# One table entry per round, the last one carried in a register, and the ring slot by modulo

## The reference

```python
# attention, per step t; x is y brought to (3072, 384)
y[t] = r[t] @ (state + (u * k[t]) outer v[t])
state = w[t][:, None] * state + k[t] outer v[t]
# layer 1: expert by normalised x against normalised expert_emb, over tau
# layer 2: expert by x @ w_gate, scaled also with sigmoid(x @ w_output_gate)
for e in range(8):
    mask = expert_idx == e
    h = np.maximum(x[mask] @ w1[e], 0.0)
    out[mask] = gate_w[mask, None] * (h @ w2[e])   # layer 2: times the output gate
```

## Time and profile before

| | |
|---|---|
| Runs | 804.28 us median of 3 (802.75 to 806.98) |
| Profiled execution | 805.82 us, of which the span is 804.1 us |
| Mean granted TensorE clock | 0.978 of full speed |
| PE busy | 734.2 us (91%) |
| PEld busy | 646.0 us (80%) |
| DVE busy | 503.9 us (63%) |
| ACT busy | 390.5 us (49%) |
| POOL busy | 161.2 us (20%) |
| HBM | 130 GB/s over the span |

### The profile page before, as it was taken

How to read it: one execution, slowest core, us unless ns; L and a number is a source line. 1 busy time by engine, 2 the same in 40 slices (tenths; PEclk the granted TensorE clock), 3 DMA queues, 4 the chain that set the end, 5 groups by cost and what they waited for, 6 DMA issues and landing times.

```text
span 804.1 us, 21458 instructions
## 1 busy us (share of the span) xinstructions
PE 734.2 (91%) x5566; PEld 646.0 (80%) x5567; DVE 503.9 (63%) x1363; ACT 390.5 (49%) x761; POOL 161.2 (20%) x202
## 2 busy tenths in 40 slices
PE   3898898883899999999999998799999999999994
PEld 2787776673788889888888887679999999999993
DVE  7889999987557574747575575544544444426621
ACT  3556767871445453636454563154444444425521
POOL 5444655554000000000000000000000000110000
PEclk9989999996999999999999999899999999999998
DMA  6655688634734251413353343233515252415110
GB/s 132 149 149 152 165 244 249 168 105 172 265 99 144 91 194 38 164 47 118 110 196 99 115 132 104 101 119 116 196 35 190 71 166 86 149 43 193 39 34 26
DMA packets 50269, 103.75 MB, mean 129 GB/s; under 512 B 7921, under 2 KB 29904, under 8 KB 50224
## 3 DMA queue, kind: packets, MB, share of 16 engines
q1 hardware_dynamic: 29536, 67.18, 26.9%
q10 hardware_dynamic: 15568, 21.76, 10.1%
q0 software_dynamic: 5120, 14.26, 4.9%
HBM read 85.73 MB, written 19.01 MB: 130 GB/s over the span
## 4 chain that ended last, share of the span: by engine, by line
PE 68%; DVE 11%; issue 7%; DMA 5%; ACT 4%; ACTq 3%; POOL 1%; SPq 1%; DVEq 0%; POOLq 0%
PE bank L1313 18%; PE bank L1339 17%; PE bank L1347 10%; PE bank L1318 9%; PE bank L1328 5%; DMA rk<-rk_in 2%; PE bank L1280 2%; PE bank L1302 2%; DVE Q L760 2%; DVE SF L769 2%; ACT wall L562 2%; PE bank L1129 1%; DMA sorted<-yrow,slot 1%; ACTq L507 1%; POOL rkp L394 1%
## 5 line engine op out<-in xcount | busy, mean ns | idle before, releaser
L1313 PE MATMUL bank<-wall,xT_hi 128*128 (+1 forms) x660 | 176.9, 403 | 1.3 <-ACT xT_hi L655 1.3
L1339 PE MATMUL bank<-wall,hT_hi 128*128 x880 | 166.9, 341 | 0.5 <-ACT hT_hi L664 0.5
L1339 PEld LDWEIGHTS bank<-wall,hT_hi 128*128 128x128 f32 x880 | 154.2, 189 | 7.9 <-issue 5.6
L875 DVE TENSOR_TENSOR wall<-raw,wall 128x1024 f32 (+1 forms) x96 | 111.9, 1220 | 62.2 <-ACT wall L562 58.9
L1313 PEld LDWEIGHTS bank<-wall,xT_hi 128*128 128x128 f32 x660 | 117.5, 188 | 21.1 <-issue 1.8
L659 ACT ACTIVATE hs<-bank 128x512 f32<-128x512 f32 x110 | 65.2, 592 | 106.7 <-PE bank L1318 106.7
L562 ACT ACTIVATE wall<-raw 128x1024 f32 (+1 forms) x96 | 95.1, 1050 | 42.4 <-issue 42.4
L664 ACT ACTIVATE hT_hi<-bank 128x512 fp32r<-128x512 f32 x110 | 59.8, 596 | 70.4 <-PE bank L1328 70.4
L1318 PE MATMUL bank<-wall,xT_lo 128*128 (+1 forms) x330 | 93.9, 392 | 0.0
L1347 PE MATMUL bank<-wall,hT_lo 128*128 x440 | 91.3, 349 | 0.0
L465 POOL DMA_INDIRECT sorted<-yrow,slot x28 | 27.4, 978 | 295.0 <-DVE yrow L1019 295.0
(11 more groups left out here) (198 smaller groups left out, 987.5 us busy)
## 6 DMA issues: line engine op xcount, KB each, us to landing
raw<-wall_in SPq DMA_DIRECT2D x96, 512.0 KB, 4.8
xin<-sorted ACTq DMA_DIRECT2D x59, 194.0 KB, 2.7
rk<-rk_in SPq DMA_DIRECT2D x46, 192.0 KB
v_in<-v_src ACTq DMA_DIRECT2D x24, 192.0 KB, 3.6
vT<-vT_in ACTq DMA_DIRECT2D x48, 96.0 KB, 4.7
wb<-w_in SPq DMA_DIRECT2D x46, 96.0 KB
sorted<-padrow SPq DMA_DIRECT2D x16, 194.0 KB, 2.3
sorted<-yrow,slot POOLq DMA_INDIRECT x28, 2.6
```

The lines of the kernel that those rows point to most:

```text
L875: v.tensor_tensor(w_lo[:, slot, cols], raw[:, q], w_hi[:, slot, cols].bitcast(F32), ALU.subtract).then_inc(w_split, 1)
L1313: pe.matmul(bank[n][:, :], xT_hi[:, k, :], w[:, bass.ds(slot, 1), cols].rearrange("p o n -> p (o n)"), start=(k == 0 and w is w_hi), stop= ...
L1339: pe.matmul(bank[2][:, 0:DM], hT_hi[:, j, :], w[:, bass.ds(slot, 1), W2 + j * DM:W2 + (j + 1) * DM].rearrange("p o n -> p (o n)"), start=( ...
```

## The change

`TAB_SLOT` and `TAB_PLACE` and the two instructions that fill them are dropped; the copy now writes the whole of `tab`. On PE the expert of tile p+1 is read once at the start of the turn and kept in the register `expert`, from which the next turn takes the expert of its tile p; the slot is the expert modulo `RING`. On ScalarE and VectorE the mark for p is read once in a turn (`following`) and kept in the register `begun`, from which the next turn takes the mark for its p-1; the place is the mark modulo `RING`. `snap` turns a register into a value that stays as it is when the register is written again, here with bounds given. The order of all other work is as it was.

```diff
@@ -50,9 +50,7 @@
 
 TAB_E, TAB_OFF, TAB_FIRST = 0, TT, 2 * TT
 TAB_LAST = TAB_FIRST + TT + 1
-TAB_SLOT = TAB_LAST + 1
-TAB_PLACE = TAB_SLOT + TT
-TAB = TAB_PLACE + TT + 1
+TAB = TAB_LAST + 1
 WRANGE = 0.25
 GT = 16
 EQ = D // 4
@@ -240,12 +238,13 @@
 
         SOON, LATE = range(3), range(3, RAWS)
 
-        def with_next_expert(eng, m, g, split, pieces):
-
-
-            e1 = eng.value_load(tab[0:1, m, bass.ds(g + TAB_FIRST + 1, 1)], min_val=0, max_val=E)
+        def following(eng, m, g):
+            return eng.value_load(tab[0:1, m, bass.ds(g + TAB_FIRST + 1, 1)], min_val=0, max_val=E)
+
+        def split_next(eng, m, g, e1, split, pieces):
+
             with eng.If(e1 > 0):
-                place = eng.value_load(tab[0:1, m, bass.ds(g + TAB_PLACE + 1, 1)], min_val=0, max_val=1)
+                place = eng.snap(e1 % RING, min_val=0, max_val=RING - 1)
                 eng.wait_ge(moes[m]["mm2"], g + 2)
                 for q in pieces:
                     split(E * m + e1, bass.ds(place, 1), q)
@@ -642,6 +641,7 @@
                 act.wait_ge(rts[1]["sel"], g)
                 act.activation(r1[:, 6:7], r1[:, 4:5], ACT.Exp, scale=-1.0).then_inc(rts[1]["ex"], 1)
 
+            begun = act.alloc_register("act_begun")
             for m in range(2):
                 mo = moes[m]
 
@@ -682,10 +682,13 @@
                     relu(0, n)
                 copy_xt(1)
                 load_rows(2)
+                act.reg_mov(begun, 0)
                 with act.Fori(0, last) as p:
                     copy_ht(p)
-                    with_next_expert(act, m, p - 1, split_hi, LATE)
-                    with_next_expert(act, m, p, split_hi, SOON)
+                    split_next(act, m, p - 1, act.snap(begun, min_val=0, max_val=E), split_hi, LATE)
+                    e1 = following(act, m, p)
+                    act.reg_mov(begun, e1)
+                    split_next(act, m, p, e1, split_hi, SOON)
                     if m == 0:
                         copy_yt(p + 1)
                         keep_row(p + 1)
@@ -697,16 +700,17 @@
                     load_rows(p + 3)
 
                 copy_ht(last)
-                with_next_expert(act, m, last - 1, split_hi, LATE)
+                split_next(act, m, last - 1, act.snap(begun, min_val=0, max_val=E), split_hi, LATE)
                 if m == 0:
-                    with_next_expert(act, m, last, split_hi, SOON)
+                    e1 = following(act, m, last)
+                    split_next(act, m, last, e1, split_hi, SOON)
                     copy_yt(last + 1)
                     keep_row(last + 1)
                     exps(last + 1)
                     copy_yt(last + 2)
                     keep_row(last + 2)
                     exps(last + 2)
-                    with_next_expert(act, m, last, split_hi, LATE)
+                    split_next(act, m, last, e1, split_hi, LATE)
 
                 act.wait_ge(mo["x_in"], 16 * last + 48)
                 part(act)
@@ -903,9 +907,7 @@
                                                 op0=ALU.is_lt, op1=ALU.mult))
                 link(v.scalar_tensor_tensor(out=FIRST, in0=NUM[:, 1:], scalar=1.0, in1=FIRST, op0=ALU.add, op1=ALU.mult))
                 link(v.tensor_scalar(tabf[:, TAB_LAST:TAB_LAST + 1], ends[:, E - 1:E], 1.0, None, ALU.subtract))
-                link(v.tensor_copy(tab[:, m, 0:TAB_SLOT], tabf[:, 0:TAB_SLOT]))
-                link(v.tensor_scalar(tab[:, m, TAB_SLOT:TAB_PLACE], tab[:, m, TAB_E:TAB_E + TT], 1, None, ALU.bitwise_and))
-                v.tensor_scalar(tab[:, m, TAB_PLACE:TAB], tab[:, m, TAB_FIRST:TAB_LAST], 1, None, ALU.bitwise_and).then_inc(tabs[m], 1)
+                v.tensor_copy(tab[:, m, :], tabf[:, :]).then_inc(tabs[m], 1)
 
             def first(u, b):
                 pre(u, b, lambda: None)
@@ -1027,6 +1029,7 @@
             link(v.tensor_copy(oha[:, 1, :], accbase[:, :]))
             v.sem_inc(r2["slots"], 1)
 
+            begun = v.alloc_register("dve_begun")
             for m in range(2):
                 mo = moes[m]
 
@@ -1066,10 +1069,13 @@
                 keep_ext(1)
                 rest_xt(1)
                 last = v.value_load(tab[0:1, m, TAB_LAST:TAB_LAST + 1], min_val=E - 1, max_val=TILES - 2)
+                v.reg_mov(begun, 0)
                 with v.Fori(0, last) as p:
                     rest_ht(p)
-                    with_next_expert(v, m, p - 1, split_lo, LATE)
-                    with_next_expert(v, m, p, split_lo, SOON)
+                    split_next(v, m, p - 1, v.snap(begun, min_val=0, max_val=E), split_lo, LATE)
+                    e1 = following(v, m, p)
+                    v.reg_mov(begun, e1)
+                    split_next(v, m, p, e1, split_lo, SOON)
                     if m == 0:
                         choose(p + 1)
                     keep_ext(p + 2)
@@ -1081,9 +1087,10 @@
                     gated(p)
 
                 rest_ht(last)
-                with_next_expert(v, m, last - 1, split_lo, LATE)
+                split_next(v, m, last - 1, v.snap(begun, min_val=0, max_val=E), split_lo, LATE)
                 if m == 0:
-                    with_next_expert(v, m, last, split_lo, SOON)
+                    e1 = following(v, m, last)
+                    split_next(v, m, last, e1, split_lo, SOON)
                     choose(last + 1)
                     place_row(last + 1)
                 v.wait_ge(mo["y_sb"], last + 1)
@@ -1096,7 +1103,7 @@
                     link(v.tensor_tensor(n_e, bank[3][:, 48:48 + E], ecap[:, :], ALU.subtract))
                     place_row(last + 2)
                     tables(1, link)
-                    with_next_expert(v, m, last, split_lo, LATE)
+                    split_next(v, m, last, e1, split_lo, LATE)
 
 
         @block.tensor
@@ -1289,12 +1296,12 @@
                     last = pe.matmul(bank[3][:, 48:48 + E], ones_r[:, :], acc, start=False, stop=True)
                 last.then_inc(r2["cnt"], 1)
 
+            expert = pe.alloc_register("pe_expert")
             for m in range(2):
                 mo = moes[m]
 
-                def weights(g):
-                    slot = pe.value_load(tab[0:1, m, bass.ds(g + TAB_SLOT, 1)], min_val=0, max_val=1)
-                    return slot, pe.value_load(tab[0:1, m, bass.ds(g + TAB_E, 1)], min_val=0, max_val=E - 1) * RAWS + E * RAWS * m
+                def weights(e):
+                    return pe.snap(e % RING, min_val=0, max_val=RING - 1), e * RAWS + E * RAWS * m
 
                 def transpose_x(g):
                     pe.wait_ge(mo["x_in"], 16 * g + 16)
@@ -1360,13 +1367,16 @@
                 pe.wait_ge(mo["xT_lo"], 1)
                 transpose_x(1)
                 last = pe.value_load(tab[0:1, m, TAB_LAST:TAB_LAST + 1], min_val=E - 1, max_val=TILES - 2)
+                pe.reg_mov(expert, 0)
                 with pe.Fori(0, last) as p:
-                    slot, pieces = weights(p + 1)
+                    old_slot, old_pieces = weights(pe.snap(expert, min_val=0, max_val=E - 1))
+                    e = pe.value_load(tab[0:1, m, bass.ds(p + TAB_E + 1, 1)], min_val=0, max_val=E - 1)
+                    pe.reg_mov(expert, e)
+                    slot, pieces = weights(e)
                     transpose_h(p)
                     first_product(p + 1, 0, slot, pieces)
                     if m == 0:
                         transpose_y(p + 1)
-                    old_slot, old_pieces = weights(p)
                     second_product_hi(p, old_slot, old_pieces)
                     if m == 0:
                         logits_y(p + 1)
@@ -1377,7 +1387,7 @@
                     second_product_lo(p, old_slot)
 
                 transpose_h(last)
-                slot, pieces = weights(last)
+                slot, pieces = weights(pe.snap(expert, min_val=0, max_val=E - 1))
                 if m == 0:
                     transpose_y(last + 1)
                     logits_y(last + 1)
```

## The result

The changed kernel takes 791.01 us as median of 6 runs (787.61 to 792.80), the kernel before 805.01 us in the 6 runs it had by then (802.75 to 806.98). The ratio is 0.9841, 95% interval 0.9816 to 0.9865, so 10.9 to 14.8 us faster. A second set of 6 runs gave 791.03 us and a ratio of 0.9828 (0.9796 to 0.9861). The forecast was 794.5 us (790.0 to 801.5), 9.8 us of gain.

What follows compares the result with a forecast made beforehand. PE was taken as bound, held in layer 1 by ScalarE's sequencer and its own reads; 4.9 + 1.9 + 1.95 + 0.5 + 0.5 + 0 = 9.8 us off the 804.3 median gives 794.5 us, range 790.0 to 801.5.

Steps and rivals of the forecast that it cites:

- The chain: Layer 1's loop: ScalarE's sequencer reads hold the first and 7 slow turns, PE's own reads stall the 18 others.
- The 7 slow turns: Layer 1 turns where an expert's SOON pieces are split, 11.56 us each: 0.7 us less a turn, 4.9 us (2.5 to 5.6).
- free pace: Layer 1 turn without stalls, taken as 10.8 us from the turn of 10.79 us with little stall.
- VectorE moves with them: Slow turns: VectorE, late next, makes the same sequencer savings and its splits follow ScalarE's; no size of its own.
- The 18 others: Layer 1's other turns, mean 10.91 us: PE's reads before L1339 go, 0.1 us a turn, 1.9 us (0 to 2.7).
- Table and entry of layer 1, with the first turn: Fewer table instructions and reads start the first turn 1.0 us earlier; it falls to 10.8: 1.95 us (0.3 to 2.6).
- End part and entry of layer 2: One mark read less on ScalarE, 0.5 us (0 to 2.2); one PE read less at entry, 0.5 (0.2 to 0.75).
- Layer 2's loop: 27 turns in which PE never idles and reads lie beside matmuls: 0 us gain.
- The bounds of a `snap`: Rival: bounds and modulo checks eat most of the reads' saving; gain 4.1 us, 800.2 us; chance 0.12.
- The raw pieces: Rival: in slow turns ScalarE starts earlier only to wait for raw pieces; that term 0, 799.4 us; chance 0.04.
- The reads were not hidden: Rival judged: reads already run beside queued engine work, so layer 1's turns stay; gain 3.0 us, 801.3 us; chance 0.03.
- The modulo: Rival: modulo is a long sequence on PE at each turn's start, slower, 839 us at 1.0 us each; chance 0.03.

## Why the prediction was right, and where it was short

- *The chain.* Right. The slow turns hung on ScalarE's sequencer (two reads put back on ScalarE bring 11.74 us back), PE's other stall on its four reads.
- *The 7 slow turns*, 4.9 us foretold with 5.6 as its upper end: 7 x (11.57 - 10.71) = 6.0. What ScalarE saves was sized right: the idle time ahead of its first split fell by 1.04 us (1.75 to 0.71) for 0.9 foretold, as the additions cost less than the 0.3 us put on them. But the sum went by what a turn can give back, 11.56 less a free pace of 10.8, and that pace was wrong. "VectorE moves with them" was right for the change as a whole, and the experiments show how much it carried: without VectorE's and PE's parts 0.24 of the 0.86 us come.
- *The 18 others*, 1.9 us foretold with 2.7 as its upper end: 18 x (10.91 - 10.71) = 3.6. This is the term that was mis-sized most, and by the same step: I took the turn of 10.79 us as PE's free pace, because it showed the smallest stall. It had one still: the weight loads of L1339 begin 3.26 us into it, 3.4 in most other turns, and 3.18 in the changed kernel (L1346), whose turns take 10.71. The row that I had would have given the size: 4.6 us of idle in 22 times is 0.21 us a turn. (The printed 18 x 0.1 stands for 18 x 0.107.)
- *TensorE's queue.* The Trainium skill ("TensorE: Matmul & The Clock Gate", section "Architectural detail: the array is 16x 32x32, not 1x 128x128") has it 64 deep, by which these reads would be hidden. With the four reads of before PE lost 0.2 us a turn in layer 1 (10.91 against 10.71), and with all four at the turn's start it waited 31.2 us in the 26 turns. The trace decides against that use of the rule in layer 1; in layer 2 the reads of before are hidden (258.8 us with four a turn, 258.9 with one).
- *Table and entry of layer 1, with the first turn*, 1.95 us foretold. From the attention's last YT to the second turn it was 219.32 - 179.4 = 39.9 us; changed, 213.47 - 174.5 = 39.0, and 214.2 - 176.5 = 37.7 in its second profile. So 0.9 and 2.2 us. In the first of them PE ran 3.4 us at a granted clock of 0.50 just there; in the profile of before and in the second one it did not. The first turn fell to 11.09 and 10.92 us, not to 10.8.
- *End part and entry of layer 2*, 0.5 + 0.5 us foretold, ends 2.2 and 0.75: 2.8 us. PE's wait for y fell from 1.96 to 1.10, 0.86; the issue ahead of layer 2's loop from 1.87 to 0.66, 1.2; both terms were about half of what came. (In the other runs with ScalarE's part the end part took 29.0, 28.5 and, with VectorE's part and three halved stretches in it, 31.0 us; with PE's part alone 30.9.) L1339's 16 products, 4.31 us before (501.15 to 505.46) with the clock halved for 2.9 us of it, took 3.06; 1.25 us that I had as the clock's upper end. It was in part given back when a halved stretch fell on layer 2's first products (L1320 at 502.48, 2.11 us for 1.6). Whether the shorter wait keeps the clock up I can't say: of the fourteen profiles with this part each has one to three halved stretches in it, at differing places.
- *Layer 2's loop*, 0 foretold: +0.1 us.
- *Rivals.* The bounds of a `snap` cost no instruction. The raw pieces were there in the slow turns; in the first turn they are now the bound. The reads were not hidden: 9.6 us came from the loop's turns after the first. But the prediction went too far where it took ScalarE's idle time as speaking against work being queued past a read: what follows ScalarE's reads in a slow turn is a branch on the value read and a split at a place from it, so nothing here shows whether work that doesn't depend on a read could pass it. The modulo adds to an address step at most some 80 ns (123 ns for 46, on PE).

Sum by stretch: 10.3 (loop, first turn with it) + 0.3 (entry) + 2.8 - 0.1 = 13.3 us against 9.8.

## What to carry to other kernels

An engine at half load can hold the chain through its sequencer: look for "issue" ahead of its first long instruction, and count reads into registers there at 0.6 to 0.75 us each; here a value worked out from one already in a register cost about a tenth of that. Several engines in one loop hold a turn one behind the other: a part tried alone may show a quarter of its worth or none, so take the next holder's part with it before you drop it. The free pace of a loop is not its best turn while every turn has some wait.

## What the runs showed of the hardware that I had not expected

What a read of a table entry by TensorE's sequencer costs depends on how many there are in a turn and where: in layer 1's turns three cost next to nothing (10.75 us for 10.71), four in two pairs 0.2 us (10.91), and the same four in a row at the turn's start 42 us over the kernel. A `snap` with bounds issued nothing. Now and then a single read took about twice the usual time, 555 ns for 288 on ScalarE. And the attention, the same work in all fourteen profiles, began its last YT anywhere from 174.5 to 180.2 us, a spread of more than most single edits here are worth.
